# A spectral filter whose way back takes one matmul: the halves of the product are swapped by ScalarE and added by VectorE

## The reference

```python
X = np.fft.rfft(x, axis=1)                      # x: 2 x 3008 x 256
Y = X * (filt_r + 1j * filt_i)[None, :, :]
y = np.fft.irfft(Y, n=3008, axis=1).astype(np.float32).reshape(6016, 256)
h = y @ moe_w_in;  g = np.where(h > 0, h, np.exp(np.minimum(h, 0)) - 1);  y = g @ moe_w_out
h = y @ moe2_w_in; g = h * np.clip(h + 3, 0, 6) / 6;                      out = g @ moe2_w_out
```

## Time and profile before

| what | us |
|---|---|
| median of 3 runs (lowest to highest) | 1127.57 (1125.98 to 1127.70) |
| the profiled execution | 1130.12 |
| its span, from the first to the last instruction | 1127.9 |
| TensorE busy | 1112.2 (99%) |
| VectorE busy | 807.2 (72%) |
| ScalarE busy | 659.5 (58%) |
| GpSimd busy | 294.6 (26%) |

### The profile page before, as it was taken

One profiled execution on the slowest core, in us unless ns is written; L12 is line 12 of the kernel. 1 busy time (PEld: TensorE's weight loads), 2 busy tenths in 40 slices (PEclk: granted clock), 3 DMA queues, 4 the chain that ended last, 5 costly groups with the idle time before them and its releaser, 6 DMA issues.

```text
span 1127.9 us, 13342 instructions
## 1 busy us (share of the span) xinstructions
PE 1112.2 (99%) x4842; PEld 892.6 (79%) x4842; DVE 807.2 (72%) x1044; ACT 659.5 (58%) x981; POOL 294.6 (26%) x228
## 2 busy tenths in 40 slices
PE   8999999999999999999999999999999999999998
PEld 4666778888888888888877788888888888888886
DVE  6777478877778778877899876666666666665655
ACT  0221456666656666666666766666665665665654
POOL 3876412202102102111278641111111111120000
PEclk9999999999999999999999999999999999999999
DMA  9887300100200200200311200200200101000000
GB/s 243 261 263 245 113 1 0 56 20 0 74 1 1 74 1 1 74 1 1 111 38 46 103 1 1 74 1 1 74 1 9 65 1 37 38 1 1 37 1 36
DMA packets 29360, 59.29 MB, mean 53 GB/s; under 512 B 3344, under 2 KB 19344, under 8 KB 29296
## 3 DMA queue, kind: packets, MB, share of 16 engines
q1 hardware_dynamic: 22960, 48.10, 13.3%
q10 hardware_dynamic: 6336, 10.36, 2.7%
HBM read 39.94 MB, written 18.51 MB: 52 GB/s over the span
## 4 chain that ended last, share of the span: by engine, by line
PE 92%; DVE 5%; ACT 1%; issue 1%; DMA 1%; SPq 0%; ACTq 0%
PE ps L383 43%; PE ps L374 13%; PE ps L373 13%; PE ps L372 13%; PE ps L340 2%; PE ps L315 2%; DVE e L610 2%; PE ps L331 2%; PE ps L332 2%; PE ps L323 2%; DVE e L608 2%; DVE g_lo L615 1%; ACT e L490 1%; DMA x_ring<-x_dev 1%; ACT w_hi L466 0%
## 5 line engine op out<-in xcount | busy, mean ns | idle before, releaser
L615 DVE TENSOR_TENSOR g_lo<-e,g_hi 128x502 fp32r<-128x502 f32 (+1 forms) x288 | 262.5, 939 | 124.1 <-ACT g_hi L520 124.1
L372 PE MATMUL ps<-op_hi,w_hi 128*128 128x502 f32 x672 | 262.4, 390 | 0.8 <-DVE h L629 0.8
L374 PE MATMUL ps<-op_lo,w_hi 128*128 128x502 f32 x672 | 262.3, 390 | 0.0
L373 PE MATMUL ps<-op_hi,w_lo 128*128 128x502 f32 x672 | 261.7, 389 | 0.0
L383 PE MATMUL ps<-g_hi,w_hi 128*128 128x502 f32 x768 | 236.7, 389 | 4.0 <-ACT g_hi L520 4.0
L383 PE MATMUL ps<-g_lo,w_hi 128*128 128x502 f32 x768 | 237.9, 391 | 2.1 <-DVE g_lo L615 1.9
L383 PE MATMUL ps<-g_hi,w_lo 128*128 128x502 f32 x768 | 235.6, 388 | 0.0
L681 POOL TENSOR_TENSOR op_lo<-op_raw,op_hi 128x1004 fp32r<-128x1004 f32 (+1 forms) x48 | 100.3, 2091 | 484.7 <-ACT op_hi L474 484.7
L383 PEld LDWEIGHTS ps<-g_hi,w_hi 128*128 128x128 f32 x768 | 143.9, 188 | 35.1 <-ACT g_hi L520 6.5
L383 PEld LDWEIGHTS ps<-g_lo,w_hi 128*128 128x128 f32 x768 | 143.8, 188 | 33.7 <-DVE g_lo L615 5.2
L383 PEld LDWEIGHTS ps<-g_hi,w_lo 128*128 128x128 f32 x768 | 144.5, 188 | 29.3
(11 more groups left out here) (51 smaller groups left out, 1173.9 us busy)
## 6 DMA issues: line engine op xcount, KB each, us to landing
f_ring<-f_dev SPq DMA_DIRECT2D x32, 384.0 KB, 4.8
op_raw<-y SPq DMA_DIRECT2D x36, 251.0 KB, 3.6
y<-ystage SPq DMA_DIRECT2D x12, 502.0 KB, 2.8
out_dev<-ystage SPq DMA_DIRECT2D x12, 502.0 KB, 2.8
x_ring<-x_dev SPq DMA_DIRECT2D x15, 384.0 KB, 6.4
y<-ystage ACTq DMA_DIRECT2D x24, 235.0 KB, 2.8
w_raw<-w_dev ACTq DMA_DIRECT2D x16, 256.0 KB, 4.2
w_raw<-w_dev SPq DMA_DIRECT2D x16, 256.0 KB, 3.1
```

The costliest lines, as they stand in the source:

```text
L372: pe.matmul(out, w_hi[p][:, cols], hi, start=start, stop=False, skip_group_check=True)
L373: pe.matmul(out, w_lo[p][:, cols], hi, start=False, stop=False, skip_group_check=True)
L374: pe.matmul(out, w_hi[p][:, cols], lo, start=False, stop=True, skip_group_check=True).then_inc(done, 1)
L615: return dve.tensor_tensor(g_lo[:, tiles, :], e[:, tiles, :], f32(g_hi[:, tiles, :]), ALU.subtract)
```

## The change

part_r becomes one matmul. What the second one did is done ahead of it: ScalarE copies the spectrum in ps to a tile swap with its two halves of 64 partitions exchanged (two copies of 64 partitions x 384 columns), VectorE multiplies swap by the filter's imaginary part in place, and adds it to prod_r. The sign's upper half is negated. I2J and prod_i go. The orders are new: TensorE does part_x(i+1) before part_a(i+2); VectorE does product_i(i), product_r(i+1), turn_a(i+2), turn_r(i); ScalarE does swap_halves(i+1) in each step behind the piece and before load_w and weight_hi. x is loaded by single groups into five slots, and the matrices in three loads. turn_r keeps its stride.

```diff
-MATS = ("A", "BX", "I2", "I2J", "I1")
+MATS = ("A", "BX", "I2", "I1")
...
-                if m >= XSLOTS:
-                    sp.wait_ge(a_done, 2 * (m - XSLOTS) + 2)
...
+                if i >= XSLOTS:
+                    sp.wait_ge(a_done, i - XSLOTS + 1)
+                sp.dma_start(x_ring[0:AROWS, i % XSLOTS],
+                             x_dev[c][:, g * GCOL:g * GCOL + GCOL]).then_inc(x_loaded[i % XSLOTS], 16)
...
             def part_x(i):
                 pe.wait_ge(spec_ready, i + 1)
                 if i >= 2:
-                    pe.wait_ge(prod_ready, i - 1)
+                    pe.wait_ge(swap_ready, i - 1)
...
-                dst = ps_r(i)[:, :, 0:K2]
-                pe.matmul(dst, mat("I2"), prod_r[:, i % 2, :], start=True, stop=False)
-                pe.matmul(dst, mat("I2J"), prod_i[:, i % 2, :], start=False, stop=True).then_inc(r_done, 1)
+                pe.matmul(ps_r(i)[:, :, 0:K2], mat("I2"), prod_r[:, i % 2, :],
+                          start=True, stop=True).then_inc(r_done, 1)
...
             for i in range(NG):
+                if i + 1 < NG:
+                    part_x(i + 1)
                 if i + 2 < NG:
                     part_a(i + 2)
-                if i + 1 < NG:
-                    part_x(i + 1)
...
+            def swap_halves(i):
+                act.wait_ge(prod_r_ready, i + 1)
+                if i >= 2:
+                    act.wait_ge(prod_ready, i - 1)
+                act.copy(swap[0:64, i % 2, :], ps_x(i)[64:P])
+                act.copy(swap[64:P, i % 2, :], ps_x(i)[0:64]).then_inc(swap_ready, 1)
+
+            swap_halves(0)
             for i in range(NG + PIECES):
                 n = piece_at(i - 1) if i <= NG else None
                 if n is not None:
                     evac_piece(n)
+                if i + 1 < NG:
+                    swap_halves(i + 1)
...
-                dve.tensor_tensor(prod_r[:, i % 2, :], ps_x(i), f_ring[:, i % FSLOTS, 0, :], ALU.mult)
+                dve.tensor_tensor(prod_r[:, i % 2, :], ps_x(i), f_ring[:, i % FSLOTS, 0, :],
+                                  ALU.mult).then_inc(prod_r_ready, 1)
+
+            def product_i(i):
+                dve.wait_ge(swap_ready, i + 1)
                 dve.wait_ge(signed, i + 1)
-                dve.tensor_tensor(prod_i[:, i % 2, :], ps_x(i), f_ring[:, i % FSLOTS, 1, :],
-                                  ALU.mult).then_inc(prod_ready, 1)
+                dve.tensor_tensor(swap[:, i % 2, :], swap[:, i % 2, :], f_ring[:, i % FSLOTS, 1, :],
+                                  ALU.mult).then_inc(prod_i_ready, 1)
+                dve.wait_ge(prod_i_ready, i + 1)
+                dve.tensor_tensor(prod_r[:, i % 2, :], prod_r[:, i % 2, :], swap[:, i % 2, :],
+                                  ALU.add).then_inc(prod_ready, 1)
...
-            products(0)
+            product_r(0)
             for i in range(NG):
+                product_i(i)
+                if i + 1 < NG:
+                    product_r(i + 1)
                 if i + 2 < NG:
                     turn_a(i + 2)
-                if i + 1 < NG:
-                    products(i + 1)
                 turn_r(i)
```

More of the change, by code:

```diff
@@ L32 @@
 NPIECE = len(ORDER) * PIECES
-XSLOTS = 4
+XSLOTS = 5
 FSLOTS = 3
 YSLOTS = 4
-MATS = ("A", "BX", "I2", "I2J", "I1")
+MATS = ("A", "BX", "I2", "I1")
 T = 502
@@ L90, in dft_matrices @@
             m["I2"][k1, s], m["I2"][64 + k1, s] = si, co
-    m["I2J"][0:64], m["I2J"][64:P] = m["I2"][64:P], -m["I2"][0:64]
     return np.stack([m[n] for n in MATS], axis=1).reshape(P, len(MATS) * P).astype(np.float32)
@@ L118, in build @@
             sign = sbuf(fft, "sign", [P, K2])
-            x_ring = sbuf(fft, "x_ring", [P, XSLOTS, 2 * GCOL])
+            x_ring = sbuf(fft, "x_ring", [P, XSLOTS, GCOL])
             f_ring = sbuf(fft, "f_ring", [P, FSLOTS, 2, XCOL])
@@ L122, in build @@
             prod_r = sbuf(fft, "prod_r", [P, 2, XCOL])
-            prod_i = sbuf(fft, "prod_i", [P, 2, XCOL])
+            swap = sbuf(fft, "swap", [P, 2, XCOL])
             back = sbuf(fft, "back", [P, 2, J, P])
@@ L161, in out_pair @@
             return ps[:, 2 * t:2 * t + 2, 0:T]
-        a_mat_loaded, mats_loaded, sign_loaded = sem("a_mat_loaded"), sem("mats_loaded"), sem("sign_loaded")
-        x_first = sem("x_first")
+        mat_loaded = {n: sem(f"mat_{n}_loaded") for n in ("A", "BX", "back")}
+        sign_loaded = sem("sign_loaded")
         x_loaded = [sem(f"x_loaded{k}") for k in range(XSLOTS)]
@@ L168, in build @@
         a_done, x_done, r_done, i_done = sem("a_done"), sem("x_done"), sem("r_done"), sem("i_done")
-        spec_ready, prod_ready, back_ready = sem("spec_ready"), sem("prod_ready"), sem("back_ready")
+        spec_ready, back_ready = sem("spec_ready"), sem("back_ready")
+        prod_r_ready, prod_i_ready, prod_ready = sem("prod_r_ready"), sem("prod_i_ready"), sem("prod_ready")
+        swap_ready = sem("swap_ready")
         signed = sem("signed")
@@ L218, in _, with load_x @@
         def _(sp):
-            def load_x(m, half=None):
-                c, g2 = ORDER[m // (GROUPS // 2)], m % (GROUPS // 2)
-                if m >= XSLOTS:
-                    sp.wait_ge(a_done, 2 * (m - XSLOTS) + 2)
[L223 to L226, removed]
+            def load_x(i):
+                c, g = group_of(i)
+                if i >= XSLOTS:
+                    sp.wait_ge(a_done, i - XSLOTS + 1)
+                sp.dma_start(x_ring[0:AROWS, i % XSLOTS],
+                             x_dev[c][:, g * GCOL:g * GCOL + GCOL]).then_inc(x_loaded[i % XSLOTS], 16)
             def load_f(i):
@@ L269, in store_out @@
                              ystage[:, t].rearrange("p (o t) -> p o t", o=2)).then_inc(y_stored[t], 16)
[L271 to L274, removed]
+            sp.dma_start(mat("A"), mats_dev[:, 0:P]).then_inc(mat_loaded["A"], 16)
+            load_x(0)
+            sp.dma_start(mat("BX"), mats_dev[:, P:2 * P]).then_inc(mat_loaded["BX"], 16)
+            load_x(1)
             sp.dma_start(sign[:], sign_dev).then_inc(sign_loaded, 16)
+            load_x(2)
             load_f(0)
-            load_x(1)
+            sp.dma_start(mats[:, 2 * P:], mats_dev[:, 2 * P:]).then_inc(mat_loaded["back"], 16)
+            load_x(3)
             load_f(1)
+            load_x(4)
             load_f(2)
-            load_x(2)
-            load_x(3)
+            for i in range(5, XSLOTS):
+                load_x(i)
             sp.wait_ge(zeroed, 2)
@@ L286, in _ @@
                     load_f(i + FSLOTS - 1)
-                if i % 2 == 0 and XSLOTS <= i // 2 + 3 < NG // 2:
-                    load_x(i // 2 + 3)
+                if i and i + XSLOTS - 1 < NG:
+                    load_x(i + XSLOTS - 1)
                 if i == 26:
@@ L307, in part_a @@
             def part_a(i):
[L308 to L312, removed]
+                pe.wait_ge(x_loaded[i % XSLOTS], 16 * (i // XSLOTS + 1))
                 if i >= 2:
@@ L315, in part_a @@
                 pe.matmul(ps_a(i), mat("A")[0:AROWS],
-                          x_ring[0:AROWS, m % XSLOTS, i % 2 * GCOL:i % 2 * GCOL + GCOL],
+                          x_ring[0:AROWS, i % XSLOTS, :],
                           start=True, stop=True).then_inc(a_done, 1)
@@ L347, in _ @@
                           start=True, stop=True)
-            pe.wait_ge(a_mat_loaded, 16)
+            pe.wait_ge(mat_loaded["A"], 16)
             part_a(0)
             part_a(1)
-            pe.wait_ge(mats_loaded, 16)
-            pe.wait_ge(zeroed, 4)
+            pe.wait_ge(mat_loaded["BX"], 16)
             part_x(0)
             for i in range(NG):
+                if i + 1 < NG:
+                    part_x(i + 1)
                 if i + 2 < NG:
                     part_a(i + 2)
-                if i + 1 < NG:
-                    part_x(i + 1)
+                if i == 0:
+                    pe.wait_ge(mat_loaded["back"], 16)
+                    pe.wait_ge(zeroed, 4)
                 part_r(i)
@@ L571, in turn_a, with product_r @@
                 dve.transpose(spec[:, i % 2, :], ps_a(i)).then_inc(spec_ready, 1)
-            def products(i):
+            def product_r(i):
                 dve.wait_ge(x_done, i + 1)
@@ L733 @@
     f_dev = np.concatenate(parts, axis=3).transpose(0, 1, 2, 3)
-    sign_dev = np.concatenate([sgn, sgn], axis=0)
+    sign_dev = np.concatenate([-sgn, sgn], axis=0)
     def pieces(w_in, w_out):
```

## The result

| | before | after |
|---|---|---|
| median of 4 runs, us | 1127.5 | 1156.6 |
| lowest to highest | 1126.0 to 1127.7 | 1153.8 to 1158.9 |
| span of the profiled execution | 1127.9 | 1151.9 |
| last turn_r starts at | 121.2 | 138.8 |
| the 64 parts of part_i behind it | 7.4 | 14.0 |

The ratio is 1.026, 95% interval 1.024 to 1.028: 29 us slower, where 14.7 were forecast and 1151 was the top of the range. The profiled execution is the fastest of the four and holds 24 of the 29 us.

What follows compares the result with a forecast made beforehand. TensorE's matmul chain bounded the transform before; afterwards VectorE, waiting for GpSimd, would. Start, seven cycles of 11.95 us and last steps put the last turn_r at 135.9 against 121.2: 1127.6 + 14.7 = 1142.3 us, range 1129 to 1151.

Steps and rivals of the forecast that it cites:

- TensorE's sum: TensorE's matmuls per loop step after the change: 2.19 us in a plain step, 3.28 with L340's parts.
- VectorE's 3.05: VectorE's instructions in one transform step after the change, without waits for GpSimd: 3.05 us.
- The turns with GpSimd: In the transform, VectorE instructions with two SBUF inputs and GpSimd instructions reading SBUF exclude each other for a whole instruction.
- Rival 1: No contention between the new VectorE instructions and GpSimd in the transform: 1119 us, or 1123 by DMA; chance 14%.
- rival 2: Turns only half as bad, GpSimd not getting in between product and addition: 1129 us; chance 14%.
- The worked cycle: Three loop steps with all GpSimd kinds take 9.15 + 2.8 = 11.95 us; seven cycles run from step 4 to 25.
- The last four steps: Loop steps 28 to 31, with GpSimd's operand sums and op_lo: last addition ends at 14.7, last turn_r starts at 135.9.
- The 64 parts of L340 behind it and all of the rest stay: After the loop's last turn_r, the 64 L340 parts and everything later keep their times, adding nothing to +14.7 us.
- the clock as a rival: TensorE's clock falls to 1.2 GHz in three to five stretches, 1.7 us lost in each: 1148 to 1151; chance 10%.
- the prediction's first step: A change of the profiled execution's span (1127.9 us) is added to the median of the runs, 1127.6.
- ScalarE, weights, DMA: In the transform, ScalarE's swaps, x and weight loads and DMA stay covered, each costing between 0 and 2 us.
- Rival 4: Late weights hold ScalarE's queue and so the swap, 1.5 us over eight loads: 1145 to 1154; chance 6%.

Runs made afterwards that it cites:

- Experiment 1: Changed kernel with ScalarE writing the exchanged halves to a PSUM bank instead of SBUF, one buffer instead of two: 1134.1 us, ratio 1.004.
- experiments 7 and 8: Changed kernel with only the swapped product (7: 1141.0 us, ratio 1.010) or only the addition (8: 1139.4 us, ratio 1.009) having two SBUF inputs.
- experiment 4: Changed kernel with GpSimd only writing zeros to w_lo in the transform instead of reading w_raw and w_hi: 1140.0 us, ratio 1.010.
- experiment 9: Changed kernel with exchange in PSUM, GpSimd's operand low parts behind all signs, unread 256-column matmuls around the last three part_r: 1124.6 us, ratio 0.997.
- experiment 10: Changed kernel, exchange still in SBUF, with unread 192-column matmuls where TensorE waits longest, in the loop and at its end: 1147.8 us, ratio 1.017.
- experiments 5 and 6: Experiment 1 plus unread 502-column matmuls around the last three part_r (5: 1127.9 us); 6 also moves GpSimd's operand low parts behind all signs (1127.8 us).
- experiment 11: Kernel before, with the last part_r also waiting until GpSimd's last low part of the operand is done: 1136.8 us, ratio 1.008.

## Why the prediction was right in its sign and wrong in its size

**TensorE's sum and VectorE's 3.05 (right).** In the changed kernel an undisturbed plain step takes 3.05 (turn_r at 15.58 and 18.63), those with a piece about 3.27. The first turn_r came at 12.35, forecast 13.2.

**The turns with GpSimd (right, and shown).** Experiment 1 removes the second SBUF input and takes away 21.8 us of the loop; experiments 7 and 8 show it for each instruction by itself, experiment 4 that GpSimd must read for it. The rule of the Trainium skill quoted in the prediction ("SBUF — State Buffer", section "Who interferes with whom") is borne out: the addition took 553 to 555 ns with one input in PSUM, 557 to 2677 with both in SBUF. Rival 1 falls with it, and rival 2 too: L680 and later op_lo did get in between product and addition.

**The worked cycle (right, with luck).** Step 25 was to start at 108.8 and started at 106.6; step 28 at 120.3, and it was 120.6. It began 1.9 earlier, with step 4 at 23.2 for 25.1, and the seven cycles took 83.5 us for a forecast of 83.7. Single ones are not alike (10.7 to 14.3 against 11.95 on paper), and 2.2 of the 83.5 are waits of VectorE for TensorE at 1.2 GHz, which were not in the working: the turns themselves were forecast 2.4 too long.

**The last four steps (2.6 too small).** Step 31's addition was to end 14.7 after step 28's start and ended at 16.5. The working let no op_lo part meet that addition; the third one started 0.04 us before it and held it for 2.1 us. The rest is part_r at 1.2 GHz, 1.65 for 0.81.

**"The 64 parts of L340 behind it and all of the rest stay" (wrong).** This is the step that failed. The 64 parts took 13.97 instead of 7.38, 6.6 us. The prediction had the clock as a rival, of a few short stretches because TensorE works only 2.2 of 4 us in a plain step. Three such stretches did come, behind steps in which an addition waited long for GpSimd, and VectorE waited for TensorE 3.7 us in all in and just behind them; most plain steps ran at 1.00 (15.4 to 37.8). What the rival did not have is the long one. The long wait that the prediction itself had worked out, TensorE without work from its last piece until the last addition, stood directly ahead of the longest row of matmuls in the transform, and it was not asked what that row would cost at the other clock. Giving the clock a chance of its own beside the forecast was the second half of the error: it was no alternative to the contention but followed from the idle time that came with it, so both had to be added.

**What separates 1142.3 from 1156.6.** The 6.6 alone would have given 1148.9. The late last turn_r, 138.8 for 135.9, adds 2.9, most of it the last four steps. The other 5 come from the prediction's first step, which carries a change of the profiled execution's span over to the median of the runs: the profile of before was of an execution 2.6 above its median, the changed kernel's own profile lies 2.8 below its, and its slower executions have a lower mean clock (0.981 to 0.985 against 0.986). By that clock the slowest spends some 10 us more at 1.2 GHz (an estimate, from 0.981 and 0.986 of 1157 us); where, no trace shows.

**The sum as the experiments leave it.** One matmul less a step, with both costs removed: -3.5 us (experiment 9). Contention: 1147.8 - 1124.6 = 23 us (experiment 10 against 9, same chip; 9 also has GpSimd's low parts later, which experiments 5 and 6 show to be worth little). Clock: ratio 1.026 - 1.017, about 10 us (changed kernel against experiment 10; on different chips, so by the ratios). Together 29, as they must, since each term starts where the other ends. Of the 10, 6.6 are seen at the 64 parts and 0.8 at part_r; the rest, some 2 to 3, is not located: the three stretches inside the loop could hold it, but between the two profiled loops it is made up again by other turns. Of the 23, some 19 were in the forecast: 14.7, and the 4.2 by which the loop ends earlier when nothing contends.

**ScalarE, weights, DMA (right).** VectorE waited 1.0 us in all for the swap, once, and ScalarE's weight_hi was never behind in a way that reached the path. Rival 4 did not happen.

## What to carry to other kernels

A VectorE instruction with both inputs in SBUF isn't of the same kind as one that reads PSUM, though both take 0.55 us alone: before moving data out of PSUM, list what GpSimd reads from SBUF in that stretch, and expect each such instruction to wait for what is left of a GpSimd instruction, and a dependent pair to let one in between. If the bank is there, put the copy in PSUM: here that alone made the loop 21.8 us shorter. And when work is taken from TensorE, look for the place where it is left with least to do, whether in one wait (3.98 us) or in two (1.90 each), and cost the matmuls behind it at 1.2 GHz, on top of the wait.

## What the runs showed of the hardware

- Once fallen, the clock stayed at 1.2 GHz for 20.5 us in one piece while TensorE was busy for 16.7 of them, on 64 parts of 94 columns with a weight load each. The same parts at 2.4 GHz didn't lower it (7.38 us, clock 1.00). In all five traces in which the row began at 1.2 GHz (the changed kernel, experiments 1, 4, 7 and 8) it ran so to its end, 13.96 or 13.97 us, so the fall nearly doubled the whole row. Between other matmuls (inside the loop, and in experiment 10) the falls lasted 3.4 us. Why the small parts don't bring the clock back is not shown.
- The same wait of TensorE (3.4 us, experiment 11) went with a lower mean clock in two of four executions. The spread of the times, 4.8 us, says nothing about it by itself: 17 executions of the kernel before on that chip spread over 4.8 too (1125.6 to 1130.4).
- A VectorE instruction with both inputs in SBUF isn't held by a GpSimd memset into SBUF (thirteen cases in experiment 4, 0.53 to 0.56 us), nor the memset by it (0.68 to 0.69).
- Two ScalarE copies of 64 partitions x 384 columns take 0.48 and 0.47 us into SBUF and 0.45 each into PSUM (experiment 1), about what a full-height copy of that width would take, an estimate from the earlier trace rows.
- The waits of the two VectorE instructions when only one has both inputs in SBUF (0.41 and 0.38) add up to those when both have (0.79).
